# Ranks of the first two chunks summed on VectorE alone, and another order of the low parts at the first experts

## What is computed

```python
def _moe2_ref(x, w_gate, w1, w2):
    N, D = x.shape                      # 1536, 512
    E = w_gate.shape[1]                 # 8
    cap = N // E                        # 192
    logits = x @ w_gate
    order = np.argsort(-logits.flatten())
    assigned = -np.ones(N, dtype=np.int64)
    counts = np.zeros(E, dtype=np.int64)
    for idx in order:
        tok, e = (int(idx) // E, int(idx) % E)
        if assigned[tok] >= 0 or counts[e] >= cap:
            continue
        assigned[tok] = e
        counts[e] += 1
    out = np.zeros((N, D), dtype=np.float32)
    for e in range(E):
        mask = assigned == e
        out[mask] = np.maximum(x[mask] @ w1[e], 0.0) @ w2[e]
    return out
```

## Time and profile before

| | |
|---|---|
| median of 3 runs | 637.48 us (636.48 to 637.87) |
| the profiled execution | 636.95 us, span 635.2 us |
| TensorE busy | 619.5 us, 98% of the span |
| VectorE busy | 394.4 us, 62% |
| GpSimd busy | 319.2 us, 50% |
| ScalarE busy | 291.8 us, 46% |

### The profile page before, as it was taken

How to read it: one execution, slowest core, us unless ns; L and a number is a source line. 1 busy time by engine, 2 the same in 40 slices (tenths; PEclk the granted TensorE clock), 3 DMA queues, 4 the chain that set the end, 5 groups by cost and what they waited for, 6 DMA issues and landing times.

```text
span 635.2 us, 13489 instructions
## 1 busy us (share of the span) xinstructions
PE 619.5 (98%) x4881; PEld 512.5 (81%) x4881; DVE 394.4 (62%) x1269; ACT 291.8 (46%) x695; POOL 319.2 (50%) x229
## 2 busy tenths in 40 slices
PE   9999999999999999999999999999989989999995
PEld 6666669989899899989997887777668878888884
DVE  6888882111124217724998998888946667676670
ACT  6899893333333332323322224243426636566541
POOL 7566663545455445444555662000092985668741
PEclk9999999999999999999999999999989989999999
DMA  9374232334454364346213151413459458866600
GB/s 292 89 298 130 77 94 67 101 102 122 147 164 130 109 191 133 102 111 216 71 34 134 52 185 48 150 51 103 182 183 408 165 188 295 286 239 228 214 25 26
DMA packets 76097, 94.38 MB, mean 149 GB/s; under 512 B 4448, under 2 KB 53888, under 8 KB 75392
## 3 DMA queue, kind: packets, MB, share of 16 engines
q1 hardware_dynamic: 73696, 86.82, 41.6%
q0 software_dynamic: 2048, 6.29, 2.9%
q10 hardware_dynamic: 288, 0.41, 0.2%
HBM read 87.16 MB, written 6.34 MB: 147 GB/s over the span
## 4 chain that ended last, share of the span: by engine, by line
PE 92%; DVE 4%; issue 2%; DMA 1%; POOL 1%; ACT 0%; POOLq 0%; DVEq 0%
PE bank L1183 14%; PE bank L1301 13%; PE bank L1185 13%; PE bank L1184 13%; PE bank L1401 9%; PE bank L1109 4%; PE bank L1170 4%; PE bank L1424 4%; PE bank L1129 4%; PE bank L1403 4%; PE bank L1195 2%; PE bank L1256 1%; PE bank L1345 1%; PE bank L1175 1%; PE bank L1123 1%
## 5 line engine op out<-in xcount | busy, mean ns | idle before, releaser
L512 POOL TENSOR_TENSOR wl_ab<-raw_ab,wh_ab 128x1024 fp32r<-128x1024 f32 x46 | 110.1, 2393 | 117.1 <-ACT wh_ab L624 117.1
L1183 PE MATMUL bank<-xh,wh_ab 128*128 128x384 f32 x384 | 133.0, 346 | 0.0
L1185 PE MATMUL bank<-xh,wl_ab 128*128 128x384 f32 x384 | 128.7, 335 | 0.0
L1184 PE MATMUL bank<-xl,wh_ab 128*128 128x384 f32 x384 | 128.6, 335 | 0.0
L894 DVE TENSOR_TENSOR hid<-hid,bank 128x384 f32<-128x384 f32 x48 | 26.6, 554 | 127.0 <-ACT hid L638 127.0
L582 POOL TENSOR_TENSOR w2l<-w_raw,w2h 128x1024 fp32r<-128x1024 f32 x32 | 75.6, 2388 | 43.9 <-DVE w1l L998 43.7
L638 ACT ACTIVATE hid<-bank 128x384 f32<-128x384 f32 x48 | 23.6, 492 | 150.1 <-PE bank L1185 150.1
L1401 PE MATMUL bank<-xg,w1h 128*128 128x384 f32 x256 | 78.8, 374 | 3.0 <-issue 2.1
L1183 PEld LDWEIGHTS bank<-xh,wh_ab 128*128 128x128 f32 x384 | 72.0, 188 | 8.9 <-issue 8.3
L872 DVE TENSOR_SCALAR_CACHE_REDUCE ge<-lb,L 128x384 bf16<-128x384 f32 (+2 forms) x72 | 72.6, 1008 | 3.3 <-PE bank L1195 3.3
L1184 PEld LDWEIGHTS bank<-xl,wh_ab 128*128 128x128 f32 x384 | 72.2, 188 | 0.0
(11 more groups left out here) (151 smaller groups left out, 1217.9 us busy)
## 6 DMA issues: line engine op xcount, KB each, us to landing
w_sb<-in_moe_w_dram SPq DMA_DIRECT2D x8, 2048.0 KB, 9.2
w_raw<-in_moe_w_dram SPq DMA_DIRECT2D x32, 512.0 KB, 8.2
raw_ab<-in_moe_w_a_dram SPq DMA_DIRECT2D x48, 256.0 KB, 2.9
raw_ab<-in_moe_w_b_dram SPq DMA_DIRECT2D x48, 256.0 KB, 3.2
raw_out<-in_moe_w_out_dram SPq DMA_DIRECT2D x24, 256.0 KB, 2.6
lb<-logit_rows SPq DMA_DIRECT2D x4, 1536.0 KB, 6.5
v_sb<-in_v_dram SPq DMA_DIRECT2D x8, 384.0 KB
woT<-in_moe_w_outT_dram SPq DMA_DIRECT2D x1, 3072.0 KB, 11.0
```

What stands on the lines that cost most here:

```text
L512: pool.tensor_tensor(wl_ab[s % 2][:, :], raw_ab[s % 3][:, :], wh_ab[s % 2][:, :].bitcast(F32), ALU.subtract).then_inc(abl_done, 1)
L1183: pe.matmul(dst, lh, rh, start=first, stop=False)
L1184: pe.matmul(dst, lh, rl, start=False, stop=False)
L1185: return pe.matmul(dst, ll, rh, start=False, stop=last)
```

## The change

It has two parts.

*Ranks.* For the six tiles of chunks 0 and 1 nothing is counted on TensorE. A new function `sum_rows` makes both directions on VectorE: the comparison with the own chunk's earlier tokens as before (mask `OWN`), one with the own chunk's later tokens (`is_le`, with a new mask `LATER` of negative ones in bank 7), and for tiles of chunk 1 both comparisons between chunk 1 and chunk 0: the tile against chunk 0, and the tile of chunk 0 against chunk 1. So a unit of chunk 0 has two instructions and one of chunk 1 has four. The sums go to `rank_parts` and a new tile `rank_more`, which one more addition joins; `base_rn` is shifted for the first chunk. The units of chunk 0 stand in the steps where its groups stood, three in a step. The 24 units of chunk 1 stand two in each of steps 28 to 35, four in step 36 and two in each of steps 38 and 39. TensorE waits for them (`row_summed`) before it writes logits into the bank of the mask, and before the first count. The groups of chunks 2 and 3 are as before.

*Low parts at the first experts.* GpSimd makes two of the four low parts of w2 of expert 1 before it waits for the low parts of expert 1's w1, not after. VectorE makes the second low part of expert 0's w1 ahead of the places, and holds the last one until the first gathered rows are there. TensorE issues four more transposes between the halves of the first `expert_in` and five after it.

```diff
+    SUMMED = 2 * TC
+    GROUPS = (NT - SUMMED) * E
+    ROWS = 2 * TC * E + 4 * TC * E
...
+    def summed_in(s):
+
+        c, f = s // NF, s % NF
+        if c == 1 and f >= F_COMPARE:
+            return [(t, f - F_COMPARE) for t in range(TC)]
+        units = {}
+        at = 0
+        for step, n in [(2 * NF + F_COMPARE + i, 2) for i in range(E)] + [(3 * NF, 4), (3 * NF + 2, 2), (3 * NF + 3, 2)]:
+            units[step] = [(TC + u % TC, u // TC) for u in range(at, at + n)]
+            at += n
+        assert at == TC * E
+        return units.get(s, [])
...
             pool.wait_ge(w1l_done, 2 * KD)
-            low_w2(1, range(4))
+            low_w2(1, range(2, 4))
...
+            def sum_rows(t, e):
...
+                if n >= 8:
+                    dve.wait_ge(row_summed, n - 4)
+                dve.scalar_tensor_tensor(out=junk[:, 0:own], in0=lb[:, c, e, 0:own], scalar=li,
+                                         in1=OWN[:, C - own:C], op0=ALU.is_ge, op1=ALU.mult,
+                                         accum_out=rank_parts[:, t, e, 1:2]).then_inc(row_summed, 1)
+                dve.scalar_tensor_tensor(out=junk[:, C:C + later], in0=lb[:, c, e, C - later:C], scalar=li,
+                                         in1=LATER[:, 0:later], op0=ALU.is_le, op1=ALU.mult,
+                                         accum_out=(rank_parts[:, t, e, 0:1] if c == 0 else rank_more[:, t, e:e + 1])
+                                         ).then_inc(row_summed, 1)
+                if c == 1:
+                    dve.tensor_scalar(junk[:, 2 * C:3 * C], lb[:, 0, e, :], li, 0.0, ALU.is_ge, ALU.add,
+                                      accum_out=rank_parts[:, t, e, 0:1]).then_inc(row_summed, 1)
+                    dve.tensor_scalar(junk[:, 3 * C:4 * C], lb[:, 1, e, :], L[:, t - TC, e:e + 1], 0.0, ALU.is_gt, ALU.add,
+                                      accum_out=rank_more[:, t - TC, e:e + 1]).then_inc(row_summed, 1)
...
             link(dve.tensor_reduce(parts[:, :, :], rank_parts[:, :, :, :], AX.X, ALU.add))
+            link(dve.tensor_tensor(parts[:, 0:SUMMED, :], parts[:, 0:SUMMED, :], rank_more[:, :, :], ALU.add))
...
-            for kk in range(1, KD):
-                low_w1(0, kk)
+            low_w1(0, 2)
+            dve.wait_ge(yg_in[0][0], 16)
+            low_w1(0, 3)
             xg_low(0)
...
-                if c > 0 and F_COMPARE <= f < F_COMPARE + E:
+                if c > 2 and F_COMPARE <= f < F_COMPARE + E:
                     for t in range(TC * (c - 1), TC * c):
                         count_group(t, f - F_COMPARE)
...
+                if c == 1:
+                    pe.wait_ge(row_summed, 2 * TC * E)
+                if c == 2:
+                    pe.wait_ge(row_summed, ROWS - 4 * 4)
...
+                    if e == 0 and h == 1:
+                        keep_clock_up(banks[7], 4)
...
             expert_in(0)
+            keep_clock_up(banks[7], 5)
```

More of the change, by code:

```diff
@@ L865, in compare @@
                 li = L[:, t, e:e + 1]
+                if m < 4:
+                    dve.wait_ge(row_summed, ROWS)
                 if m >= 4:
@@ L880, in compare_of_step @@
                 c, f = s // NF, s % NF
-                if c > 0 and F_COMPARE <= f < F_COMPARE + E:
-                    if c == 1 and f == F_COMPARE and k == 0:
-                        dve.wait_ge(parts_cleared, 1)
-                        dve.wait_ge(mask_up, 1)
+                here = summed_in(s)
+                if k == 0 and here and here[0][1] == 0 and here[0][0] % TC == 0:
+                    dve.wait_ge(parts_cleared, 1)
+                    dve.wait_ge(mask_up, 1)
+                    dve.wait_ge(later_up, 2)
+                    dve.wait_ge(lb_in[c - 1], 16)
+                    dve.wait_ge(l_out, c)
+                if s == 3 * NF + 2 and k == 0:
+                    dve.wait_ge(l_ready, c)
+                for unit in here[k:k + 1] if k < 2 else here[2:]:
+                    sum_rows(*unit)
+                if c > 2 and F_COMPARE <= f < F_COMPARE + E:
                     if f == F_COMPARE and k == 0:
@@ L1005, in _ @@
             low_w1(0, 0)
+            low_w1(0, 1)
             dve.wait_ge(pos_ready, 1)
@@ L1189, in count_group @@
                 m = group_of(t, e)
-                if t >= TC:
-                    pe.wait_ge(ge_ready, rows_before(m + 1))
+                if m == 0:
+                    pe.wait_ge(row_summed, ROWS)
+                pe.wait_ge(ge_ready, m + 1)
                 pe.wait_ge(ge_diag, m + 1)
```

41 lines of the change are left out of this document (26 added, 15 removed).

## The result

The changed kernel takes 629.51 us (median of 4 runs, 628.32 to 630.48) beside 637.67 us for the kernel before on the same chip: a ratio of 0.987, 95% interval 0.985 to 0.990. In a second comparison it took 629.39 beside 636.20 us, ratio 0.989 (0.987 to 0.991). The forecast was 625.2 us with an own range of 624.3 to 626.2, and 629.5 as the upper end of everything that it allowed for. So it is faster, as forecast, but by two thirds of the gain, outside the own range and at the very edge of the wide one. The profiled execution took 630.48 us, its span is 628.8 us; the second comparison's has a span of 626.9 us.

What follows compares the result with a forecast made beforehand. TensorE was taken as the bound, 92% of the chain of waits. Terms of 6.3 + 0.5 + 1.5 + 3.9 = 12.2 us off 636.95 gave 624.8, forecast as 625.2 us (own range 624.3 to 626.2, wide 623.6 to 629.5).

Steps and rivals of the forecast that it cites:

- Term A: Gated stage: taking the counts of chunks 0 and 1 off TensorE gains 6.3 us, 5.3 to 6.5.
- VectorE's lag: Chunk 1's steps: VectorE falls behind by 2.9 us in all, within its slack, so TensorE does not stall.
- Term B: First gather: with only one low part behind the indices, 0.5 us gained, the middle of 0 and 1.0.
- The cover: Before the first gather: the store of y hides the 1.16 us low part moved ahead, with 0.9 us to spare.
- Term C: After the first gather: added transposes keep TensorE's clock up, gaining 1.5 us, bounds 0 and 1.5.
- rival 1: After the first gather: the clock falls anyway, by idling or because transposes don't hold it; 626.7 us, chance 0.20.
- Term D: Third expert (e = 2): moving two of GpSimd's four w2 low parts earlier gains 3.9 us, 0 to 4.2.
- The collision at expert 2: GpSimd still splits when VectorE starts its w1 low parts, so the expert takes 4.2 us too long; all taken as gone.
- Its price at expert 1: Expert 1: GpSimd's moved pair may block VectorE's low part for 0.3 us, where TensorE has no slack.

Runs made afterwards that it cites:

- e7: The changed kernel with GpSimd subtracting only half the columns of each gated weight block; 627.44 us in a single profiled execution.
- e11: The changed kernel with the two wide sums of each row of chunk 1 cut from 384 to 64 columns; 628.37 us in a single profiled execution.
- e6: The changed kernel with VectorE's low parts of expert 0's w1 in the order of before, filler transposes kept; 629.78 us, ratio 0.990.
- e4: The changed kernel without the nine filler transposes around the gather of expert 0; 628.85 us, ratio 0.989.
- e3: The kernel before with only the new order of low parts and the nine filler transposes, comparisons as before; 633.31 us, ratio 0.9946.
- e5: The changed kernel with GpSimd's four w2 subtractions for expert 1 kept together behind VectorE's w1 low parts, as before; 631.32 us, ratio 0.992.
- e2: The kernel before with only the comparisons of the first two chunks summed along rows, low parts and fillers as before; 632.35 us, ratio 0.9935.
- e9: The changed kernel with w1 of expert 1 loaded in the stage of the y products, at round 19 of 24; 626.54 us, ratio 0.9845.
- e8: The changed kernel with w1 of expert 1 asked for once expert 0's gather has landed, ahead of w2 of expert 1; 632.06 us, ratio 0.9925.

## Why the prediction was off, by its steps

**Term A** (forecast 6.3 us, own bounds 5.3 to 6.5). TensorE lost its counts and nothing else stood there, as forecast; the sums of VectorE were free, as forecast, even at step 36. From step 12 to 47 the profile gains 5.4 us (169.63 to 164.19). What was mis-sized is the period of a step without counts: it was taken from one pair of rows, 4.16 us, when such steps are 4.22 in the mean (4.16 and 4.29 in turn, or evenly). Sixteen steps times 0.06 us is 1.0 us. By stage: steps 17 to 25 gained 1.9 us (37.93 to 36.01) where 2.4 were forecast, steps 29 to 38 gained 3.6 (44.67 to 41.10) where 3.9 were. e7 shows what the floor of 4.22 is: with half of GpSimd's subtraction the same stretch gains 6.5 us over the kernel before (169.63 to 163.09), the whole of the term. VectorE's lag was free, as forecast (e11); its rate was forecast a little too high, since `hid` was counted with its duration (0.56 us) and not with the distance to the next start (0.47).

**Term B** (0.5 us, 0 to 1.0). The first gather took 2.03 us against 2.50 in the kernel before, so 0.5 us is what the rows show, but that the middle was right is luck. The question behind it has an answer: the gather was blocked, not just slow, since in every profile it ends 1.06 or 1.07 us after VectorE's low part (e6). What the forecast missed is that the one low part left behind the indices blocks it too, else it would take 0.9 us. By e6 the order of the low parts is worth 1.3 us in the gather (3.32 to 2.03) and 0.6 us at the first w1 matmul; the wide fillers, now in the path, take the rest. The cover was thinner than forecast: VectorE's indices, not the store, now release the gather.

By the rule of the Trainium skill (SBUF — State Buffer, "Who interferes with whom") a `tensor_tensor` does not hold up descriptor writing; the 1.07 us in every profile speak against that here.

**Term C** (1.5 us, with 0 as rival 1, chance 0.20). The first profile showed the clock at 1.00 through the gather, which looks like a hit, but e4 shows the same without the transposes, and they cost 0.4 us of path. They were not needed: the idling that they were to fill was gone. The half clock also did not go away, it moved: to the fillers in front of the gathered rows (second profile, e3, e5; the idling ahead of the indices that the forecast had named as the danger), or to expert 1's new waits (first profile, e6). Of the eight executions of the changed kernel two have a mean granted clock of 0.998; of 35 executions of the kernel before eight have 0.997 or more. So C brought little of its 1.5 us, how much exactly no run says, and rival 1 had the right mechanism in part.

The Trainium skill's rule (TensorE: Matmul & The Clock Gate, "Part 4: PE-mode transpose"), that transposes do not count as activity in the same way, gave 0 for this term, and e4 is with it as to the time. As to the mechanism it is open: e4 had no gap long enough to lose the clock, and e6 beside e2 (clock kept with transposes, lost without, one profile each) speaks for the forecast.

**Term D** (3.9 us, 0 to 4.2). The collision at expert 2 and its removal are as forecast, 4.2 us; e5 shows that the moved pair does it. Its price at expert 1 was forecast as 0.3 us, through VectorE. In the changed kernel it does not show, since the wait for w1 holds VectorE back longer; with that wait gone (e9) it is there, 0.4 us, as forecast.

**What the sum left out, the step that failed.** B, C and D all count work on the engines, and the forecast never asked when w1 of expert 1 lands: it put this wait at nothing without a reason. Its chain does not run through TensorE: gather of expert 1 landed, four transfers of w2, one of w1, on full DMA engines. In every profile in which ScalarE waits for it, `w1h` starts 23.9 to 24.9 us after the first gather. The compute side wanted it after 21.0 to 21.6 where no filler ran at half clock (e4, and the changed kernel's 24.70 less its wait of 3.11). In the kernel before it was in after 22.26 us and ScalarE came after 22.88: the slack was 0.6 us, and B and C together were to bring 2.0. So the forecast's 20.9 us could not be reached with this transfer where it was. The rest of the wait is the last of its sixteen parts: in the changed kernel fifteen are in after 22.28 us, the last after 24.68. The half clock at expert 1 then comes on top in some executions, 1.6 us.

In the forecast's own columns the changed kernel's span is 5.9 us over its 622.9: 0.6 in front of the gather, 3.8 from there to `w1h` (3.1 of it this wait, 0.4 the filler transposes), 1.4 at expert 1 (the half clock, less the 0.3 that did not show), 0.1 behind. With the transfer moved (e9) the stretch behind the gather is 21.36 us and the span 625.0, 2.1 over: 1.4 in front of the gather, 0.5 behind it, 0.2 at the experts. The 1.4 are a gated stage that starts 1.2 us later, term A's 0.9, and 0.7 the other way, by which the gather starts sooner, counted from step 47, than before.

For these 0.7 us the trace has a like picture: the last store of y takes 2.9 us to land in the kernel before, fifteen of its parts 0.9 us sooner than the last, with an instruction load (1.4 us) beside it; in e2 it takes 2.0 us and has no such load. What stays open is whether these loads are the cause, here and at w1. That they start 9 to 15 us behind the gather in all twelve profiles with the first part of the change, and in neither of the two without it, fits a TensorE program with fewer instructions in front, but no run tests it.

## What to carry to other kernels

Before an edit that brings compute forward, list for each later consumer the transfer that it needs, when that lands, and what the transfer itself waits for: a chain that does not pass through the busy engine does not get shorter with it, and the gain ends at its landing. A transfer lands with the last of its parts, so look at all sixteen: the slack here was 0.6 us, and one late part cost 2.4. Load a block as soon as its place is free, not when its turn in a queue comes; beside an indirect gather, though, a large load cost more than it brought here (e8). Take the floor of a loop from a mean over an even number of periods: one row of an alternating pair was worth 1 us here. And ask at whose starts you read it: VectorE's own pitch stayed at 4.21 us in e7 while TensorE ran at 4.16.

## What the runs showed that was not expected

A 2 MB transfer beside the gather of expert 1 made it land 4.8 us later (469.1 in e8 against 464.3 in e9), though the DMA engines moved only 61 to 168 GB/s there without it, of the 400 that they reach. TensorE idled for 1.36 us in e6, with transposes in the gaps behind, and kept its clock at 1.00; in the kernel before 1.35 us of idling, and 0.43 and 0.90 behind it, stood ahead of a half clock. A profile with one such dip is no proof that each execution has it: of the two profiles of the changed kernel one has it at expert 1, the other in front of the gathered rows.

One transfer of 16 KB, for instructions, goes with a last part of a 2 MB load that is 0.9 to 2.4 us late, in nine profiles of ten. And an indirect gather ends 1.07 us after VectorE's subtraction of two SBUF tensors, in 14 profiles of 14.
